# Normalising an attention tile in three passes, each counted, and one wait per transpose round

## The chip, the cores and the metric

The kernel runs on one core of a Trainium2 chip. The metric is the time on the device in microseconds, a median over several runs. The engines of a core run side by side and meet only at semaphores: PE (matmuls and transposes; its weight loads are listed apart as PEld), ACT (activations and copies), DVE (elementwise work and reductions), POOL (elementwise work, here also some DMAs) and SP (issues DMAs).

## What is computed

Three layers follow one another: attention over 16 heads with pooled queries, a mixture of four experts, and a mixture of eight experts with one expert for each token. Only the attention is touched by the change:

```
B, H, S, D = 2, 8, 1152, 64
q_pool = q.reshape(B, H, S // 2, 2, D).mean(axis=3)          # 576 queries a head
scores = scale * q_pool @ k^T                                # 576 x 1152
attn = exp(scores - max(scores))
attn = attn / (sum(attn) + 1e-9)                             # the step that is changed
out = attn @ v                                               # 576 x 64, float32
```

All is float32. To keep accuracy with the faster matmul type, operands are split in a high part (a copy in fp32r) and a low part (the rest), and products are summed over both.

## The kernel before

The 576 queries of a head are cut in five tiles (`QT`): four of 128 queries and one of 64. The 16 heads go by in eight pairs, ten tiles a pair (`TPP = 10`, `TPH = 5`); tile k of pair j has the running number g = 10 j + k, and t = k mod 5 is its place in its head. Pairs 1 to 6 are a loop on each engine, pairs 0 and 7 are written out.

For each tile: PE makes the scores (`score_tile`, L290 and L291, 128 x 1152 in three PSUM banks). DVE takes the negated row maximum (`max_tile`, L745). ACT makes the exponential and the row sum into the SBUF tile `a[t]` (`exp_tile`, L550). DVE adds 1e-9 and takes the reciprocal (`rinv_tile`, L751 and L754). POOL multiplies the whole tile by it, in place, in one instruction of 1152 columns (`norm_tile`, L1021), and raises `norm_ready` by one. PE then transposes the tile in nine blocks of 128 columns, three to a round (`transpose_round`, L307 and L309, `RPT = 3` rounds of `KPR = 3` blocks), each round into one of two PSUM banks (`ring`). ACT copies a round to `aTh` (`split_hi`, L514), DVE subtracts to `aTl` (`split_lo`, L700), and PE multiplies by V (`times_v`, L322) in two groups a head, at t = 3 (first 288 queries) and at the next head's t = 0 (the other 288).

The order is written out by hand in a function `pair` on every engine, by fixed leads: in the stage of tile k PE makes the scores of tile k + 4, ACT the exponential of k + 3, DVE the reciprocal and POOL the multiply of k + 2 (`N_LEAD = 2`), while PE, ACT and DVE transpose and split tile k. PE's order in a stage is: round 0, then `times_v` where it is due, round 1, the scores and round 2 (round 2 before the scores where `times_v` is due).

Beside the tiles, POOL makes the low parts of K and V for later heads: `sub_k` (L1006, 64 x 1152) after the multiply of the stages k = 3 and k = 8, and `sub_v` (L1012, 128 x 576) after that of k = 4 and k = 9. So four POOL instructions stand in a row: the multiply for the next head's tile 0, `sub_k`, the multiply for its tile 1, `sub_v`. SP loads a later head's K, Q and V when `k_lo`, `v_lo` and `q_sum` have risen.

DVE at k = 0 and k = 5 makes, between its splits, the low part of the scaled queries of the next head (`prep_ql`, L738, a SCALAR_TENSOR_TENSOR with both inputs in SBUF), and at k = 5 of pairs 1 to 7 it also splits the last pair's output (`split_x`: L774, a copy `xTh<-y` listed as CAST, and L700, `xTl<-y,xTh`, with two SBUF inputs). In pair 7 there is no `prep_ql` at k = 5 and no `sub_k`.

`at_least(eng, s, v)` is a `wait_ge` that is left out when v is the constant 0. Where an instruction has one wait it carries it; a further wait is an instruction of its own on the engine's queue (EVENT_SEMAPHORE in the trace), and in a loop the value waited for is made by a register operation (ALU_OP).

Of the kernel before, what the change touches and what calls it, by code (L numbers as in the profile page):

```python
# [5 lines left out]
ALU = mybir.AluOpType  # L6
# [6 lines left out]
P = 128  # L13
BATCH, HEADS, SEQ, DH = 2, 8, 1152, 64
POOL = 2
QS = SEQ // POOL
NH = BATCH * HEADS
# [3 lines left out]
TPH = len(QT)  # L21
TPP = 2 * TPH
RPT = 3
KPR = KT_N // RPT
# [29 lines left out]
def attention_moe_moe_kernel(nc, kT, qT, vr, dom, w1, w2, emb, tau, v1, v2, rows, out):  # L54
# [9 lines left out]
    def sb(name, shape, dt=F32, scope=ctx):  # L64
        return scope.enter_context(nc.sbuf_tensor(name, shape, dt))
# [4 lines left out]
    def sem(name):  # L70
        return ctx.enter_context(nc.semaphore(name))
# [3 lines left out]
    def at_least(eng, s, value):  # L75

        if not isinstance(value, int) or value > 0:
            eng.wait_ge(s, value)

    with ctx:  # L80
# [37 lines left out]
        a = [sb(f"a{i}", [P, SEQ], F32, att) for i in range(TPH)]  # L118
# [8 lines left out]
        rinv = sb("rinv", [P, TPH], F32, att)  # L127
# [65 lines left out]
        def bank(turn):  # L193
            return ring[turns.index(turn) % 2]
# [8 lines left out]
        def bank_free(eng, j, turn, first):  # L203

            i = turns.index(turn) - 2
            if first and i == turns.index(("V", 0, 1)):
                i -= 2
            if i >= 0 or not first:
                at_least(eng, *taken(j if i >= 0 else j - 1, turns[i]))
# [10 lines left out]
        S = {n: sem(n) for n in names}  # L220
# [57 lines left out]
        def _(pe):  # L278
# [15 lines left out]
            def transpose_round(t, k, r, j, g, first):  # L294

                m = QT[t][1]
                if r == 0:
                    pe.wait_ge(S["norm_ready"], g + 1)
                bank_free(pe, j, ("T", k, r), first)
                for i in range(KPR):  # L300
                    kt = KPR * r + i
                    o = bank(("T", k, r))[:, i * m:(i + 1) * m]
                    src = a[t][0:m, kt * P:(kt + 1) * P]
                    if m < P and i == 0:


                        last = pe.matmul(o, src, ident[0:m, 0:m], start=True, stop=True)  # L307
                    else:
                        last = pe.transpose(o, src, ident[0:m, 0:m])  # L309
                last.then_inc(S["t_ready"], 1)  # L310
# [46 lines left out]
            def pair(j, first, last):  # L357
                for k in range(TPP):
                    s, t = k // TPH, k % TPH
                    g = TPP * j + k  # L360
                    transpose_round(t, k, 0, j, g, first)
                    if t == 0 and not (first and k == 0):
                        times_v(2 * j + s - 1, 1 - s, 1, j, k, first)
                    if t == V_TILES[0]:
                        times_v(2 * j + s, s, 0, j, k, first)
                    transpose_round(t, k, 1, j, g, first)
                    if t in V_TILES:
                        transpose_round(t, k, 2, j, g, first)
                    if not (last and k + S_LEAD >= TPP):
                        s2, t2 = (k + S_LEAD) // TPH, (k + S_LEAD) % TPH  # L370
                        score_tile(2 * j + s2, s2 % 2, t2, g + S_LEAD)
                    if t not in V_TILES:
                        transpose_round(t, k, 2, j, g, first)
                    if last and k == TPP - 2:
                        pe.wait_ge(S["x_lo"], PAIRS - 1)
                    if last and k >= TPP - 2:

                        for f in range(2 * (k - TPP + 2), 2 * (k - TPP + 2) + 2):
                            up_tile(0, 0, f)
# [601 lines left out]
        def _(pool):  # L981
# [19 lines left out]


            def sub_k(n, s, norms):
                at_least(pool, S["norm_ready"], norms)
                pool.wait_ge(S["k_hi"], n + 1)
                pool.tensor_tensor(KT[s][DH:P, :], rawK[s][DH:P, :], KT[s][DH:P, :].bitcast(F32),  # L1006
                                   ALU.subtract).then_inc(S["k_lo"], 1)

            def sub_v(n, s, norms):
                at_least(pool, S["norm_ready"], norms)  # L1010
                pool.wait_ge(S["v_hi"], n + 1)
                pool.tensor_tensor(VV[s][:, :, DH:2 * DH], rawV[s][:], VV[s][:, :, 0:DH].bitcast(F32),  # L1012
                                   ALU.subtract).then_inc(S["v_lo"], 1)

            def norm_tile(t, g, ks, vs):
                pool.wait_ge(S["k_lo"], ks)
                pool.wait_ge(S["v_lo"], vs)
                at_least(pool, S["norm_ready"], g)
                pool.wait_ge(S["rinv_ready"], g + 1)
                m = QT[t][1]  # L1020
                pool.tensor_tensor(a[t][0:m, :], a[t][0:m, :], rinv[0:m, t:t + 1].to_broadcast([m, SEQ]),  # L1021
                                   ALU.mult).then_inc(S["norm_ready"], 1)


            pool.wait_ge(S["fill_ready"], 1)
# [9 lines left out]
            chain(pool.tensor_scalar(first1[:], prefer[:], float(E2), None, ALU.is_ge))  # L1035

            sub_v(0, 0, 0)
            pool.wait_ge(S["v_lo"], 1)
            pool.wait_ge(S["k_lo"], 1)
            sub_k(1, 1, 0)  # L1040
            for t in range(N_LEAD):
                norm_tile(t, t, 2, 1)
            def pair(j, first, last):
                for k in range(TPP):
                    s, t = k // TPH, k % TPH
                    g = TPP * j + k
                    n = 2 * j + s
                    if not (last and k + N_LEAD >= TPP):
                        norm_tile((k + N_LEAD) % TPH, g + N_LEAD, NH if last else n + 2 + (t > 3),
                                  n + 1)  # L1050
                    if t == V_TILES[0] and not last:
                        sub_k(n + 2, s, g + N_LEAD + 1)
                    if t == 4 and not (last and s == 1):
                        sub_v(n + 1, 1 - s, g + N_LEAD + 1)
# [4 lines left out]
            pair(PAIRS - 1, False, True)  # L1059

            pool.wait_ge(S["x_lo"], PAIRS)
            pool.wait_ge(S["norm_ready"], TPH * NH)
            pool.memset(acc[:], 0.0).then_inc(S["acc_zero"], 1)


# [64 lines left out]
```

## Time and profile before

| | us |
|---|---|
| median of 3 runs | 1005.42 (1002.42 to 1006.47) |
| span of the profiled execution, first to last instruction | 1002.8 |
| median less that span | 2.6 |
| PE busy in the span | 879.9 (88%) |
| DVE busy | 511.9 (51%) |
| ACT busy | 435.0 (43%) |
| POOL busy | 285.1 (28%) |
| loop pairs 1 to 6 and their neighbours, 92 to 348 us | 256.0 |

The record gives the profiled execution its span alone; its whole time on the device is not listed beside the three runs. A row of a timeline gives start, duration, engine, line, operation, output and inputs, shapes and count; the bracket at its end is the idle time of the engine before it and what ended it. Busy engines are not by themselves the limit: in the attention stages the engines hand work on in a ring, and the chain of waits says which hand-over was last.

### The profile page before, as it was taken

Reading aid. Unit: us, or ns where it says so; the run is one execution under the profiler, and the core shown is the slowest. Engines: PE = TensorE matmul, PEld = TensorE weight load, DVE = VectorE, ACT = ScalarE, POOL = GpSimd, SP = SyncE. Lnnn points to the kernel's source line nnn. Section 1 sums busy time; section 2 is a strip of 40 time slices with the busy share of each in tenths; the row PEclk is TensorE's granted clock in tenths of the full one; section 3 lists DMA queues with packets and bytes.
Section 4 is the critical chain, followed back from the end, with each engine's and each line's share of the span. In section 5 each row is a group of like instructions: output and inputs, shape, how many; then the busy total and the mean of one; then the engine's idle time right before and its main releaser. Section 6 shows DMA issues by size and latency. Waiting matters only on the chain.

```text
span 1002.8 us, 14755 instructions
## 1 busy us (share of the span) xinstructions
PE 879.9 (88%) x4740; PEld 753.5 (75%) x4741; DVE 511.9 (51%) x901; ACT 435.0 (43%) x794; POOL 285.1 (28%) x166
## 2 busy tenths in 40 slices
PE   2888888888888879999999999999999709999996
PEld 2666666666666768898989898989898607878885
DVE  4788888888878854141414141314131322299225
ACT  4677777777777643030303031303131502278224
POOL 3766667766667521000000000000000040133112
PEclk9999999999999979999999999999999858999998
DMA  8333222234227221010201120012000062197510
GB/s 263 83 83 84 71 59 59 59 81 95 59 59 185 75 85 52 33 49 37 84 1 32 53 84 0 22 62 84 1 1 1 0 235 70 42 308 255 209 42 23
DMA packets 30095, 79.66 MB, mean 79 GB/s; under 512 B 4008, under 2 KB 4008, under 8 KB 30065
## 3 DMA queue, kind: packets, MB, share of 16 engines
q1 hardware_dynamic: 27104, 70.58, 23.9%
q0 software_dynamic: 2960, 8.68, 2.7%
q8 instruction: 19, 0.31, 0.1%
q14 instruction: 12, 0.09, 0.0%
HBM read 69.52 MB, written 10.78 MB: 80 GB/s over the span
## 4 chain that ended last, share of the span: by engine, by line
PE 76%; ACT 7%; issue 6%; DVE 6%; DMA 3%; POOL 1%; SPq 1%; ACTq 0%; POOLq 0%; DVEq 0%
PE L L337 20%; PE L L400 20%; PE ring L322 7%; PE L L505 7%; PE L L479 6%; PE ring L309 4%; PE scores L290 4%; PE scores L291 3%; ACT a L550 2%; DVE aTl L700 2%; ACT aTh L514 2%; PE ring L307 1%; DMA xr<-sorted_rows 1%; ACT o_vl L514 1%; POOL sorted_rows L1069 1%
## 5 line engine op out<-in xcount | busy, mean ns | idle before, releaser
L1021 POOL TENSOR_TENSOR a<-a,rinv 128x1152 f32<-128x1152 f32 (+1 forms) x80 | 168.5, 2106 | 106.2 <-DVE rinv L754 104.1
L700 DVE TENSOR_TENSOR aTl<-ring,aTh 128x384 fp32r<-128x384 f32 (+1 forms) x240 | 118.5, 512 | 62.0 <-ACT aTh L514 60.6
L309 PE MATMUL ring<-ident,a 128*128 128x128 f32 (+1 forms) x672 | 110.4, 277 | 37.1 <-ACT o_vl L514 18.2
L514 ACT ACTIVATE aTh<-ring 128x384 fp32r<-128x384 f32 (+1 forms) x240 | 106.5, 458 | 70.9 <-PE ring L309 66.3
L619 ACT ACTIVATE hh<-L 128x384 fp32r<-128x384 f32 x96 | 46.6, 491 | 204.2 <-PE L L337 204.2
L337 PE MATMUL L<-xTh,w1h 128*128 128x384 f32 x384 | 131.2, 342 | 4.4 <-DVE hl L832 2.3
L337 PE MATMUL L<-xTl,w1h 128*128 128x384 f32 x384 | 130.8, 341 | 0.0
L337 PE MATMUL L<-xTh,w1l 128*128 128x384 f32 x384 | 130.6, 340 | 0.0
L1069 POOL DMA_INDIRECT sorted_rows<-acc,posi x9 | 10.7, 1186 | 415.0 <-DVE posi L924 412.6
L309 PEld LDWEIGHTS ring<-ident,a 128*128 128x128 f32 (+1 forms) x672 | 75.4, 145 | 64.9 <-DVE aTl L700 32.8
L832 DVE SCALAR_TENSOR_TENSOR hl<-L,hh 128x384 fp32r<-128x384 f32 x96 | 52.8, 557 | 125.4 <-ACT hh L619 125.4
L400 PE MATMUL L<-w2h,hh 128*128 128x512 f32 x288 | 114.2, 396 | 0.0
L400 PE MATMUL L<-w2l,hh 128*128 128x512 f32 x288 | 113.8, 395 | 0.0
L400 PE MATMUL L<-w2h,hl 128*128 128x512 f32 x288 | 113.7, 395 | 0.0
L745 DVE TENSOR_REDUCE negmax<-scores 128x1 f32<-128x1152 f32 (+1 forms) x80 | 107.9, 1350 | 2.2 <-PE scores L291 2.2
L839 DVE SCALAR_TENSOR_TENSOR acc<-L,pw,acc 128x512 f32<-128x512 f32 x36 | 27.0, 751 | 158.7 <-PE L L400 158.7
L290 PE MATMUL scores<-KT,QTh 128*128 128x384 f32 (+1 forms) x240 | 90.6, 378 | 13.8 <-DVE QTl L738 7.8
L550 ACT ACTIVATE a<-scores,negmax 128x1152 f32<-128x1152 f32 (+1 forms) x80 | 97.1, 1214 | 5.3 <-DVE negmax L745 5.3
L322 PE MATMUL ring<-aTh,VV 128*128 128x288 f32 x288 | 81.5, 308 | 19.1 <-DVE aTl L700 19.1
L291 PE MATMUL scores<-KT,QTl 128*128 128x384 f32 (+1 forms) x240 | 83.0, 346 | 0.0
L514 ACT ACTIVATE w2h<-raw 128x1024 fp32r<-128x1024 f32 x40 | 39.5, 1048 | 90.5 <-PE L L400 88.0
L322 PE MATMUL ring<-aTl,VV 128*128 128x288 f32 x288 | 78.5, 298 | 0.0
(155 smaller groups left out, 1580.6 us busy)
## 6 DMA issues: line engine op xcount, KB each, us to landing
raw<-in_v SPq DMA_DIRECT2D x48, 512.0 KB, 5.9
raw<-in_w SPq DMA_DIRECT2D x32, 512.0 KB, 5.2
rawK<-in_kT SPq DMA_DIRECT2D x32, 288.0 KB, 5.1
rawQ<-in_qT SPq DMA_DIRECT2D x32, 288.0 KB, 5.8
sorted_rows<-filler SPq DMA_DIRECT2D x19, 257.0 KB, 9.4
rawV<-in_vr SPq DMA_DIRECT2D x16, 288.0 KB, 5.9
xr<-sorted_rows POOLq DMA_DIRECT2D x15, 257.0 KB, 3.0
out<-o,destc POOLq DMA_INDIRECT x13, 2.8
```

Source lines behind the costliest of these rows:

```text
L290: pe.matmul(o, QTh[s][:, q0:q0 + m], KT[s][:, keys], start=True, stop=False)
L291: last = pe.matmul(o, QTl[s][:, q0:q0 + m], KT[s][:, keys], start=False, stop=True)
L309: last = pe.transpose(o, src, ident[0:m, 0:m])
L322: last = pe.matmul(O[:, 0:w], VV[s][:, kt, :], src[:, kt, q0:q0 + w], start=(kt == 0 and i == 0), stop=(kt == KT_N - 1 and i == 1))
L337: last = pe.matmul(L1[i % L1_BANKS][:, 0:CW], w[:, d, wf], x[:, cols], start=(n == 0), stop=(n == 3 * DT - 1))
L400: last = pe.matmul(L2[tt % L2_BANKS][:], h[c % 2][:, f, cols], w[:, f, :], start=(n == 0), stop=(n == 3 * FT - 1))
L505: last = pe.matmul(L2[1][:], h[:, f, :], w[:, f, :], start=(n == 0), stop=(n == 3 * FT - 1))
L514: return act.activation(o, i, ACT.Copy, **kw)
L550: act.activation(a[t][0:m, :].rearrange("p (c k) -> p c k", c=SC), scores[b][0:m, :, 0:SW], ACT.Exp, bias=negmax[0:m, t:t + 1], accum_out= ...
L700: return dve.tensor_tensor(o, i0, i1, op)
L745: dve.reduce_max(negmax[0:m, t:t + 1], scores[b][0:m, :, 0:SW], axis=AX.XY, negate=True).then_inc(S["max_ready"], 1)
L1021: pool.tensor_tensor(a[t][0:m, :], a[t][0:m, :], rinv[0:m, t:t + 1].to_broadcast([m, SEQ]), ALU.mult).then_inc(S["norm_ready"], 1)
```

## The change

POOL's multiply of a tile is issued as three instructions of 384 columns, in the order of the rounds, each raising `norm_ready` by one. Every transpose round waits for its own count instead of round 0 alone waiting for the whole tile. All other waits on `norm_ready` are scaled by `RPT = 3`, so they wait for the same event as before.

```diff
@@ transpose_round (PE)
-                if r == 0:
-                    pe.wait_ge(S["norm_ready"], g + 1)
+                pe.wait_ge(S["norm_ready"], RPT * g + r + 1)
                 bank_free(pe, j, ("T", k, r), first)
@@ sub_k, sub_v (POOL)
-                at_least(pool, S["norm_ready"], norms)
+                at_least(pool, S["norm_ready"], RPT * norms)
@@ norm_tile (POOL)
-                at_least(pool, S["norm_ready"], g)
+                at_least(pool, S["norm_ready"], RPT * g)
                 pool.wait_ge(S["rinv_ready"], g + 1)
                 m = QT[t][1]
-                pool.tensor_tensor(a[t][0:m, :], a[t][0:m, :], rinv[0:m, t:t + 1].to_broadcast([m, SEQ]),
-                                   ALU.mult).then_inc(S["norm_ready"], 1)
+                for r in range(RPT):
+                    keys = slice(r * KPR * P, (r + 1) * KPR * P)
+                    pool.tensor_tensor(a[t][0:m, keys], a[t][0:m, keys],
+                                       rinv[0:m, t:t + 1].to_broadcast([m, KPR * P]),
+                                       ALU.mult).then_inc(S["norm_ready"], 1)
@@ before the memset of acc (POOL)
-            pool.wait_ge(S["norm_ready"], TPH * NH)
+            pool.wait_ge(S["norm_ready"], RPT * TPH * NH)
```

## Rows read from the trace of the kernel before

**Rows 1.** Busy time by stretch, columns engine by engine, with instructions, clock, DMA.
```profile
92.00:348.00 256.00, 213.61 (x1365) 173.61 (x1365) 213.12 (x401) 190.46 (x382) 175.32 (x84) 1.00 0.34 83
```
**Rows 2.** Waits, 92 to 350 us: engine, line, releaser, total, times, longest.
```profile
POOL a L1021 <- DVE rinv L754: 76.3, 49, 2.8
```
**Rows 3.** Timeline, stage k = 2 of a loop pair: weight loads of transposes, POOL.
```profile
204.98 2.11 POOL L1021 TENSOR_TENSOR a<-a,rinv 128x1152 f32<-128x1152 f32 x1 [2.09 <-DVE rinv L754]
...
208.15 0.31 PEld L309 LDWEIGHTS ring<-ident,a 128*128 128x128 f32 x3 [0.15 <-DVE aTl L700]
```
**Rows 4.** Chain of waits, stage k = 5: start, duration, piece.
```profile
219.26 0.58 ACT QTh L514
...
220.54 1.68 DVE xTh L774
...
222.33 0.76 DVE xTl L700
```
**Rows 5.** Timeline of DVE, stage k = 5.
```profile
219.86 0.76 DVE L738 SCALAR_TENSOR_TENSOR QTl<-qs,QTh 128x576 fp32r<-128x576 f32 x1
220.54 1.66 DVE L774 CAST xTh<-y 128x576 f32 x1
222.33 0.76 DVE L700 TENSOR_TENSOR xTl<-y,xTh 128x576 f32 x1
```
**Rows 6.** Timeline of POOL, the four in a row, and the next multiply.
```profile
212.75 2.11 POOL L1021 TENSOR_TENSOR a<-a,rinv 128x1152 f32<-128x1152 f32 x1 [2.24 <-DVE rinv L754]
215.02 2.64 POOL L1006 TENSOR_TENSOR KT<-rawK,KT 64x1152 fp32r<-64x1152 f32 x1 [0.16 <-POOL a L1021]
217.82 2.11 POOL L1021 TENSOR_TENSOR a<-a,rinv 128x1152 f32<-128x1152 f32 x1 [0.16 <-POOL KT L1006]
220.00 1.88 POOL L1012 TENSOR_TENSOR VV<-rawV,VV 128x576 fp32r<-128x576 f32 x1
223.43 2.11 POOL L1021 TENSOR_TENSOR a<-a,rinv 128x1152 f32<-128x1152 f32 x1 [1.54 <-DVE rinv L754]
```
**Rows 7.** Timeline, stage k = 0: POOL, then DVE behind it.
```profile
198.40 1.42 POOL L1012 TENSOR_TENSOR VV<-rawV,VV 128x576 fp32r<-128x576 f32 x1
...
198.82 1.61 DVE L738 SCALAR_TENSOR_TENSOR QTl<-qs,QTh 128x576 fp32r<-128x576 f32 x1
```
**Rows 8.** Timeline of DVE, first aTl after it in stage k = 0.
```profile
201.23 1.17 DVE L700 TENSOR_TENSOR aTl<-ring,aTh 128x384 fp32r<-128x384 f32 x2 [0.53 <-ACT aTh L514]
```
**Rows 9.** All instructions of line 774: count, shortest/median/longest ns.
```profile
L774 DVE CAST xTh<-y x8: 452/1664/1664, 92.2 to 385.3; 128x576 f32 x6, 128x576 fp32r<-128x576 f32 x2
```
**Rows 10.** times_v at k = 5 and k = 8: chain in pair 0, timeline in a loop pair.
```profile
47.94 2.65 PE ring L322 x18
...
60.24 2.63 PE ring L322 x18
...
218.19 0.40 PE L322 MATMUL ring<-aTh,VV 128*128 128x288 f32 x1 [0.41 <-DVE aTl L700]
...
231.32 0.39 PE L322 MATMUL ring<-aTh,VV 128*128 128x288 f32 x1 [0.78 <-DVE aTl L700]
```
**Rows 11.** Timeline of POOL, small instructions at the start.
```profile
0.42 0.10 POOL L1119 MEMSET const-float32-0.0<- 128x1 f32 x1 [0.42 <-issue]
0.45 0.10 POOL L1119 MEMSET const-float32-1.0<- 128x1 f32 x1
...
4.78 0.24 POOL L1035 TENSOR_SCALAR first<-prefer 128x8 f32<-128x8 f32 x1
```
**Rows 12.** Sequencer work of line 1019, a wait of POOL: ns.
```profile
L1019 POOLq ALU_OP  x60: 32/32/32, 71.6 to 324.4; - x60
L1019 POOLq EVENT_SEMAPHORE  x20: 43/43/43, 24.5 to 357.5; - x20
```
**Rows 13.** Timeline of pair 7, stage k = 5: POOL's sub_v and DVE's copy.
```profile
347.58 1.43 POOL L1012 TENSOR_TENSOR VV<-rawV,VV 128x576 fp32r<-128x576 f32 x1
...
348.08 1.25 DVE L774 CAST xTh<-y 128x576 fp32r<-128x576 f32 x1
```

More of the change, by code:

```diff
@@ L1009, in sub_v @@
             def sub_v(n, s, norms):
-                at_least(pool, S["norm_ready"], norms)
+                at_least(pool, S["norm_ready"], RPT * norms)
                 pool.wait_ge(S["v_hi"], n + 1)
```

## The prediction

> **What bounds the kernel now.** I read the busy shares, then the waits, then the chain, then the timelines of the places where the chain touches POOL. In the loop pairs no engine is full: in 256.0 us PE is busy 213.6, DVE 213.1, ACT 190.5, POOL 175.3 [rows 1]. So the attention is bound by hand-overs between PE, ACT and DVE. POOL is not in that ring as a releaser: among the waits of this stretch it waits for DVE's reciprocal, 49 times, 76.3 us in all [rows 2], and no row has PE or PEld waiting for POOL. The tightest place is stage k = 2 to 3: the multiply of tile 3 runs from 204.98 to 207.09 and its first transposes load at 208.15, released by DVE's aTl [rows 3]. That leaves 1.06 us of slack. At k = 6 it ends at 219.93 [rows 6] and round 0 follows only behind xTl, which ends at 223.09 [rows 5].
>
> There is one place where POOL does reach the chain, by another way. At k = 5 of pairs 1 to 7 the chain runs ACT's QTh copy, DVE's xTh copy (1.68 us), DVE's xTl [rows 4]. That copy takes 0.45 us with POOL idle and 1.66 in the median [rows 9]. In the loop it starts at 220.54, POOL's sub_v ends at 221.88 [rows 6], and the copy ends 0.32 later, at 222.20 [rows 5]. The copy is held until POOL's instruction is over. The same happens to the SCALAR_TENSOR_TENSOR of line 738: 0.76 us where it starts ahead of sub_v [rows 5], 1.61 where sub_v (198.40 to 199.82) is running, ending 0.61 after it [rows 7]. The other way round, sub_v takes 1.42 alone [rows 7] and 1.88 behind line 738 [rows 6]. So these instructions and POOL's take turns at something, and the one that comes second waits.
>
> **The change, part by part.**
>
> Earlier release of round 0, removed wait. Gain 0: round 0 now needs only the first third of a multiply that was ready 1.06 us ahead at its tightest place [rows 3]. The cover is DVE's aTl that frees the bank; rounds 1 and 2 come later still, so a last pass that ends some tenths later is hidden too.
>
> Two more POOL instructions a tile. The trace has no multiply of 384 columns. What a further pass costs: the 1152-column sub_k takes 2.64 and the 576-column sub_v 1.42 [rows 6, 7]; the slope leaves 2.64 - 2 x (2.64 - 1.42) = 0.20 us that does not depend on the columns. An 8-column instruction takes 0.24 and a one-column memset 0.10 [rows 11]. Against that, instructions with no wait between them overlap: the memsets of 0.10 start 0.03 apart [rows 11]. I take 0.20 less some 0.07 of overlap a pass, so a multiply grows by e = 2 x 0.13, say 0.25 us, from 2.11 to 2.36. The lower end is 0: the columns are the same, so less than one instruction's time is excluded, and full overlap gives no more than that. The upper end is a fixed 0.24 with a gap of 0.16 as stands ahead of sub_k [rows 6], e = 0.8.
>
> POOL's busy time rises by 80 x 0.25 = 20 us; nearly all of it falls in idle time before a reciprocal (1.5 to 2.2 us each) [rows 6]. SP's loads start up to 0.5 later, from about 222.1; K is first copied at about 232 and a transfer of this kind lands in some 6 us, so they stay hidden.
>
> The four in a row at k = 3 and 4. Two multiplies, sub_k and sub_v run back to back with gaps of 0.16 and 0.07 [rows 6], so sub_v starts 2e = 0.50 later: 220.50. Line 738 is issued at 219.86. Now the last pass of the multiply (219.66 to 220.43) is running, so it is held 0.5 us and ends near 220.43 + 0.61 = 221.04. Sub_v has waited since 220.50 and goes next; today it ends 1.26 after line 738 does (221.88 against 220.62) [rows 5, 6], so now at 222.30. The copy ends 0.32 later, 222.62, against 222.20: +0.42. All of it goes on through xTl to the splits, since DVE is the chain there [rows 4]. That DVE's work at k = 5 is really paid for shows in the pairs: from times_v of k = 5 to that of k = 8 it takes 12.30 us in pair 0, which has no split_x, and 13.13 in a loop pair [rows 10]. The 0.83 between them is also the most that could be won here.
>
> Six loop pairs: 6 x 0.42 = 2.5 us. Pair 7 has no sub_k and no line 738; there sub_v (347.58) is behind one multiply, moves by e, and the copy, which ends 0.32 after it, moves too [rows 13]: +0.25. At k = 0 the same shift lets line 738 in ahead of sub_v or leaves it behind; it is done by 200.9 at worst, and DVE then had 0.53 idle ahead of its next split [rows 8]. Cost 0.
>
> Here the Trainium skill speaks: its page "SBUF — State Buffer", section "SBUF: two separate sides", says that VectorE and GpSimd share a port pair under an exclusive lock that the first to start holds for the whole instruction, and that VectorE takes it in its two-port modes and also with two SBUF inputs against a GpSimd op that reads SBUF. The first half agrees with the 1.66 against 0.45 us above. The second half would also hold xTl (two SBUF inputs), which no row shows next to a POOL instruction; what hangs on that is the second case below.
>
> 160 more waits on PE, for rounds 1 and 2. The nearest rows are a wait of 43 ns and a register operation of 32 on POOL's queue [rows 12]. All exposed: 160 x 0.075 = 12 us. Behind such a wait stand the round's loads, then ACT's split. I take 0: the count is long reached, and PE's queue is fed while it still works on scores or times_v or stands at a bank. Round 0 carries the same pair of waits today and starts 0.15 us after its release [rows 3]. The upper end is 4 us, one exposed wait in three.
>
> Sum: +2.5 + 0.25 = +2.8 us on a span of 1002.8. The median of the runs is 1005.4, 2.6 above the span, and I add to the median: 1008.2, 0.3% more.
>
> **The rivals.**
>
> A, nothing moves. If the passes overlap fully (e near 0), sub_v stays where it is: 1005.4. For: overlapped starts [rows 11]. Against: those are memsets that read nothing.
>
> B, faster: DVE slips in between passes. With e over about 0.43 (0.5, say) the last pass would start after line 738 is issued; line 738 goes between passes two and three and ends near 220.7, the last pass ends at 221.35 and the copy, already waiting, goes ahead of sub_v and ends at 221.67. If xTl is not held by POOL it ends at 222.56 instead of 223.09, -0.53 in six pairs; in pair 7 the copy wins against sub_v and saves 0.8: 1005.4 - 4.0 = 1001.4. If xTl is held, it waits for sub_v to end near 222.97 and the pair loses 0.5 again. Against it: line 738, with two SBUF inputs, is held [rows 7], and e must be double my value. With the 0.83 of [rows 10] in seven pairs it can't go below 999.6.
>
> C, slower: passes cost 0.97 us each, e = 0.8. Then the last pass runs to about 222.0, sub_v after the copy to 223.75, and xTl, held, to 224.36 instead of 223.09: 6 x 1.27 + 0.8 = 8.4, 1013.8. It decides at the four in a row, from e of about 0.5 on. For: the 0.24 of an instruction with 8 columns. Against: the 0.20 of the slope.
>
> D, slower: PE's waits show, up to 4 us on top of 2.8: 1012.2. Against: round 0's start today.
>
> **How the numbers follow.** Forecast (1008.2, e of 0.1 to 0.45) 0.54; A 0.14; B 0.12; C 0.12; D 0.08. A measurement of this kernel can tell about 0.5%, 5 us, from no change. B is at most 6 us, so three quarters of it count as faster: 0.09. C and D count as slower: 0.20. The rest, 0.71, is within. The range leaves out the end of B below 1001.5 and the worse part of C above 1012.5.
>
> **What would show it.** A pass should take 0.75 to 0.85 us and a multiply 2.3 to 2.5 from first start to last end. PE should wait nowhere for POOL. In the loop pairs sub_v should start about 0.5 later behind its reciprocal, line 738 at k = 5 take about 1.2 instead of 0.76, and the copy still end 0.3 after sub_v. From times_v of k = 5 to k = 8 should come 13.5 instead of 13.13, and the rest of a pair stay. I am wrong if the copy goes ahead of sub_v, if the gaps ahead of rounds 1 and 2 grow, or if the expert stages move.

## The result, and the profile after

The changed kernel takes 1009.7 us in the median of 10 runs (1007.9 to 1010.9), against 1005.2 of the kernel before in the same session. The ratio is 1.0047, 95% interval 1.0034 to 1.0059: slower by 4.5 us (3.4 to 5.9), where the prediction had 2.8.

The page of the changed kernel, its head. POOL has 160 instructions more and is 27.1 us longer busy (24.3 in the multiplies, 2.7 in sub_v; forecast 20). No other engine has more work, but PE's queue has 195 waits and register operations more, which the page doesn't count as busy.

```profile
span 1006.6 us, 15170 instructions
...
PE 879.1 (87%) x4740; PEld 752.0 (75%) x4741; DVE 510.2 (51%) x901; ACT 435.1 (43%) x794; POOL 312.2 (31%) x326
```

Most of the loss is in the loop pairs. Below are the first times_v instructions of k = 0, 3, 5, 8 and of the next pair's k = 0, in the timeline of the changed kernel (start, duration, engine, line, operation; in brackets the idle time before). The rows that answer to the third and the fourth are the last two of [rows 10].

```profile
200.34 0.40 PE L321 MATMUL ring<-aTh,VV 128*128 128x288 f32 x1 [0.42 <-DVE aTl L699]
...
212.88 0.37 PE L321 MATMUL ring<-aTh,VV 128*128 128x288 f32 x1 [0.89 <-DVE aTl L699]
...
221.48 0.37 PE L321 MATMUL ring<-aTh,VV 128*128 128x288 f32 x1 [0.43 <-DVE aTl L699]
...
235.26 0.37 PE L321 MATMUL ring<-aTh,VV 128*128 128x288 f32 x1 [0.80 <-DVE aTl L699]
...
243.85 0.40 PE L321 MATMUL ring<-aTh,VV 128*128 128x288 f32 x1 [0.42 <-DVE aTl L699]
```

The same of the kernel before, at k = 0, 3 and the next 0; k = 5 (218.19) and k = 8 (231.32) are the rows named above.

```profile
197.16 0.40 PE L322 MATMUL ring<-aTh,VV 128*128 128x288 f32 x1 [0.42 <-DVE aTl L700]
...
209.57 0.39 PE L322 MATMUL ring<-aTh,VV 128*128 128x288 f32 x1 [0.88 <-DVE aTl L700]
...
239.95 0.40 PE L322 MATMUL ring<-aTh,VV 128*128 128x288 f32 x1 [0.42 <-DVE aTl L700]
```

| stretch, us | before | changed | difference |
|---|---|---|---|
| k = 0 to 3 | 12.41 | 12.54 | +0.13 |
| k = 3 to 5 | 8.62 | 8.60 | -0.02 |
| k = 5 to 8 | 13.13 | 13.78 | +0.65 |
| k = 8 to 0 | 8.63 | 8.59 | -0.04 |
| a loop pair | 42.79 | 43.51 | +0.72 |

Six pairs make 4.3 us; from the first of them at k = 3 to the same place in pair 7 it is 4.5 (256.6 before, 261.1 changed). The rest of the spans' difference of 3.8 us is small and of both signs: by the same starts, 0.56 before the first times_v of k = 3, 0.50 in pair 0, and then -1.0 in the last pair and -0.7 in the experts. The 0.56 can't be put down to the change: in the profiled executions of all nine kernels this first stretch takes 39.3 to 41.2 us, and experiment 5, which has the code of before there, takes 40.97. The -1.0 is probably no merit of the change either. These are the stretches from pair 7's k = 3 to the last times_v (time, then busy times, then the granted clock, DMA share and GB/s). The first row is before, the second after. The profiled execution of before spent more of it at the lower of the two clock levels, 1.2 GHz (0.88 of full speed in the mean, against 0.92), and PE took 1.2 us longer over the same 188 instructions. That the clock makes the whole difference is not shown: the kernel of experiment 6 takes 41.0 there at 0.92.

```profile
337.85:379.32 41.47, 33.20 (x188) 28.87 (x189) 23.65 (x43) 20.49 (x42) 13.06 (x7) 0.88 0.16 52
```

```profile
343.40:383.84 40.44, 32.00 (x188) 27.64 (x189) 24.20 (x43) 20.50 (x42) 15.73 (x18) 0.92 0.16 53
```

**POOL and DVE at k = 5.** The timeline of the changed kernel; it answers to [rows 5 and 6].

```profile
218.60 2.64 POOL L1005 TENSOR_TENSOR KT<-rawK,KT 64x1152 fp32r<-64x1152 f32 x1 [0.16 <-POOL a L1022]
...
221.40 2.40 POOL L1022 TENSOR_TENSOR a<-a,rinv 128x384 f32<-128x384 f32 x3 [0.16 <-POOL KT L1005]
...
223.13 1.28 DVE L737 SCALAR_TENSOR_TENSOR QTl<-qs,QTh 128x576 fp32r<-128x576 f32 x1
...
223.88 1.80 POOL L1011 TENSOR_TENSOR VV<-rawV,VV 128x576 fp32r<-128x576 f32 x1
...
224.34 1.66 DVE L773 CAST xTh<-y 128x576 f32 x1
...
226.12 0.76 DVE L699 TENSOR_TENSOR xTl<-y,xTh 128x576 f32 x1
```

Three passes take 2.40 us together where one took 2.11. Line 737 (738 before) is now issued while the last pass runs and takes 1.28 instead of 0.76; before, it was issued 0.07 before the multiply ended and so hardly waited. It ends 0.61 after the last pass; sub_v waits for it; the copy is held until sub_v ends at 225.68 and ends 0.32 later, as before. Counted from times_v of k = 5, xTl ends at 5.40 (226.88 - 221.48) instead of 4.90 (223.09 - 218.19): +0.50.

**PE's waits.** The timeline of the kernel before, one freed bank at k = 7: aTl ends at 227.75, the weight load starts at 227.80.

```profile
227.19 0.56 DVE L700 TENSOR_TENSOR aTl<-ring,aTh 128x384 fp32r<-128x384 f32 x1 [0.44 <-ACT aTh L514]
...
227.80 0.31 PEld L309 LDWEIGHTS ring<-ident,a 128*128 128x128 f32 x3 [0.95 <-DVE aTl L700]
```

The same place in the changed kernel: aTl ends at 231.60, the load starts at 231.72.

```profile
231.04 0.56 DVE L699 TENSOR_TENSOR aTl<-ring,aTh 128x384 fp32r<-128x384 f32 x1 [0.50 <-ACT aTh L513]
...
231.72 0.31 PEld L308 LDWEIGHTS ring<-ident,a 128*128 128x128 f32 x3 [1.01 <-POOL a L1022]
```

Take the transposes' loads between 92 and 348 us that PE waited for and that start less than 160 ns after the end of an aTl: the median distance went from 53 ns (67 loads) to 116 (83 loads). The sequencer's records of line 78, the function that waits for a bank, show why. Before (from 92 to 348 us; count, duration in ns):

```profile
L78 PEldq ALU_OP  x163: 32/32/36, 93.4 to 322.2; - x163
...
L78 PEldq EVENT_SEMAPHORE  x10: 51/51/51, 324.0 to 346.4; - x10
```

After:

```profile
L78 PEldq EVENT_SEMAPHORE  x168: 51/51/51, 92.6 to 347.0; - x168
L78 PEldq ALU_OP  x66: 32/32/36, 92.8 to 327.7; - x66
```

Of the two waits of a round, the first-written one (the count, long reached) is now carried by the weight load, and the bank's, which really ends last, has become an instruction of 51 ns in front of it. The trace lists the semaphore of each wait and bears this out: between 92 and 318 us the transposes' loads carry the wait on `norm_ready` 130 times in the changed kernel and never before, and the register operations that carried it before (53 times, round 0's) carry it 26 times. The bracket "<-POOL a L1022" in the row at 231.72 is a trap: the load carries the wait on POOL's count, and so the record names POOL. Wherever it does so, the tile's last pass had ended at least 1.9 us before. From 92 to 350 us the changed kernel's list of waits puts 16.3 us (25 waits) down to POOL for the loads of line 308 and 3.0 us (12 waits) for those of line 306, and none of it is time that POOL cost.

### The profile page after: what moved, and what is told of

The parts are those of the page before. It is cut to its first block, busy times and chain, and to the rows that moved or that the text cites. A ratio compares the mean times of both kernels' runs of the same rounds, so it can differ in the third digit from the quotient of the medians.

```text
span 1006.6 us, 15170 instructions
## 1 busy us (share of the span) xinstructions
PE 879.1 (87%) x4740; PEld 752.0 (75%) x4741; DVE 510.2 (51%) x901; ACT 435.1 (43%) x794; POOL 312.2 (31%) x326
## 4 chain that ended last, share of the span: by engine, by line
PE 78%; DVE 7%; ACT 5%; issue 5%; DMA 3%; POOL 1%; SPq 1%; ACTq 0%; POOLq 0%; DVEq 0%
PE L L336 20%; PE L L399 20%; PE L L504 7%; PE ring L321 6%; PE L L478 6%; PE ring L308 6%; PE scores L290 5%; PE scores L291 4%; DVE aTl L699 3%; ACT aTh L513 2%; PE ring L306 1%; DMA xr<-sorted_rows 1%; POOL sorted_rows L1071 1%; PE L L486 1%; DVE xTh L773 1%
## 5 line engine op out<-in xcount | busy, mean ns | idle before, releaser
L1022 POOL TENSOR_TENSOR a<-a,rinv 128x384 f32<-128x384 f32 (+1 forms) x240 | 192.8, 831 | 85.8 <-DVE rinv L753 81.9
```

The costliest lines, as they stand in the source:

```text
L1022: pool.tensor_tensor(a[t][0:m, keys], a[t][0:m, keys], rinv[0:m, t:t + 1].to_broadcast([m, KPR * P]), ALU.mult).then_inc(S["norm_ready"], 1)
```

## The experiments

The theory has two parts: POOL's longer multiply pushes sub_v and with it DVE's copy (the port part, after the port pair that the prediction cites for the two engines' taking turns), and the bank's wait now costs an instruction on PE (the wait part). The rivals are either of them alone.

**1. PE's waits alone.** One multiply as before, all else as in the change.

```diff
-                for r in range(RPT):
-                    ...
+                pool.tensor_tensor(a[t][0:m, :], a[t][0:m, :], rinv[0:m, t:t + 1].to_broadcast([m, SEQ]),
+                                   ALU.mult).then_inc(S["norm_ready"], RPT)
```

> One multiply of 1152 columns as before, raising the count by 3; PE waits in every transpose round as in the change. Theory 1 (two causes: the port shift through POOL's longer multiply, and a wait instruction on PE's queue that now stands between the freed bank and the transposes): a round starts 0.12 us after DVE's aTl instead of 0.05, a loop pair takes 42.79 + 0.20 to 0.25 us, the copy xTh ends where it did; about +1.5 to +2 us in all. Theory 2 (POOL alone): a loop pair stays at 42.79 and the time at that of before. Theory 3 (PE's waits alone are the whole loss): a pair takes 43.5 and the time is +4.5.

Measured: 1007.7 against 1004.7, ratio 1.0027 (1.0016 to 1.0037). The five times_v starts of its timeline, k = 0, 3, 5, 8, 0:

```profile
200.16 0.40 PE L321 MATMUL ring<-aTh,VV 128*128 128x288 f32 x1 [0.41 <-DVE aTl L699]
...
212.70 0.37 PE L321 MATMUL ring<-aTh,VV 128*128 128x288 f32 x1 [0.89 <-DVE aTl L699]
...
221.31 0.37 PE L321 MATMUL ring<-aTh,VV 128*128 128x288 f32 x1 [0.42 <-DVE aTl L699]
...
234.62 0.37 PE L321 MATMUL ring<-aTh,VV 128*128 128x288 f32 x1 [0.80 <-DVE aTl L699]
...
243.21 0.39 PE L321 MATMUL ring<-aTh,VV 128*128 128x288 f32 x1 [0.41 <-DVE aTl L699]
```

A pair takes 43.05, +0.26: 0.13 in k = 0 to 3, 0.18 in k = 5 to 8, and a few hundredths less in the other two. That is four times the 0.06 by which a round starts later; for the other rounds of a pair it doesn't show. The median distance from aTl to load is 115 ns. Waits alone cost, so theory 2 falls. The medians differ by 3.0 us (1.6 to 3.7), above the expected 1.5 to 2; the trace has 2.1 of it between pair 0's k = 3 and pair 7's.

**2. POOL's passes alone.** The change with PE waiting once a tile.

```diff
-                pe.wait_ge(S["norm_ready"], RPT * g + r + 1)
+                if r == 0:
+                    pe.wait_ge(S["norm_ready"], RPT * (g + 1))
```

> Three passes of 384 columns as in the change, but PE waits once for all three, in round 0 alone, as before. Theory 1: sub_v starts 0.58 us later, xTl ends 0.50 later, a loop pair takes 42.79 + 0.50 = 43.3, with all of it between times_v of k = 5 and of k = 8; rounds start 0.05 after DVE's aTl; +3 us. Theory 2: all of the loss, a pair at 43.5, +4.5. Theory 3: nothing.

Measured: 1007.3, ratio 1.0029 (1.0017 to 1.0042). Its times_v starts at k = 0, 3, 5, 8, 0:

```profile
198.58 0.39 PE L322 MATMUL ring<-aTh,VV 128*128 128x288 f32 x1 [0.41 <-DVE aTl L700]
...
210.98 0.40 PE L322 MATMUL ring<-aTh,VV 128*128 128x288 f32 x1 [0.88 <-DVE aTl L700]
...
219.62 0.40 PE L322 MATMUL ring<-aTh,VV 128*128 128x288 f32 x1 [0.41 <-DVE aTl L700]
...
233.23 0.40 PE L322 MATMUL ring<-aTh,VV 128*128 128x288 f32 x1 [0.79 <-DVE aTl L700]
...
241.85 0.39 PE L322 MATMUL ring<-aTh,VV 128*128 128x288 f32 x1 [0.41 <-DVE aTl L700]
```

A pair takes 43.27, +0.48, all of it between k = 5 and k = 8 (13.61); k = 0 to 3 stays at 12.40, and the distance from aTl to load is back at 53 ns. The two parts add up: 0.26 + 0.48 = 0.74 a pair, against 0.72 in the changed kernel. PE here waits for the last pass in round 0, and nothing is late for want of an earlier count: in the loop pairs round 0 starts 0.7 us or more after its tile's last pass. The medians can't show this sum: +3.0 and +2.6 make 5.6 against 4.5, with intervals of some 1 us to either side of each. It rests on the times_v starts, which agree from one loop pair to the next within 0.04 us.

**3. The waits in the other order.**

```diff
-                pe.wait_ge(S["norm_ready"], RPT * g + r + 1)
                 bank_free(pe, j, ("T", k, r), first)
+                pe.wait_ge(S["norm_ready"], RPT * g + r + 1)
```

> The changed kernel with the two waits of a transpose round written in the other order, the bank first and the count second. If the delay on PE comes from which wait is carried by the weight load and which is an instruction of its own ahead of it, the bank's wait now is carried, rounds start 0.05 us after DVE's aTl again, and a loop pair takes 43.3 instead of 43.5: about -1.5 us against the change. If the delay comes from the number of wait and register instructions, it stays at 43.5.

Measured: 1008.4, ratio 1.0037 (1.0022 to 1.0051). Half of the expectation came. In pair 0, where the counts are constants, the median distance is 53 ns again and k = 5 to 8 takes 12.32, against 12.52 in the changed kernel and 12.30 before. These are its times_v pieces of pair 0 in the chain of waits (k = 5 and 8), to set beside the first two of [rows 10]:

```profile
48.20 2.65 PE ring L321 x18
...
60.52 2.62 PE ring L321 x18
```

In the loop it didn't help: 123 ns and 43.66 in the pair from 200.11, no better than 43.51. The sequencer's records of line 298, the count's wait, say how:

```profile
L298 PEldq ALU_OP  x110: 32/32/32, 92.1 to 329.3; - x110
L298 PEldq FUSED_REGOPS  x54: 37/37/51, 96.5 to 327.1; - x54
L298 PEldq EVENT_SEMAPHORE  x13: 51/51/51, 329.7 to 347.1; - x13
```

In the loop the count's value is made by a register operation, which stands between the two waits; in the records that operation itself carries the bank's wait, and the load comes behind it, so the freed bank still has another instruction to release first. So it is not the number of waits but which instruction the last-ending one sits on.

**4. Nine passes.** POOL's part in a larger dose, PE waiting once.

```diff
-                for r in range(RPT):
+                for c in range(KT_N):
                     ...                                 # 128 columns each
```

> Nine passes of 128 columns, PE waiting once in round 0 as before: a larger dose of the POOL part. A pass more costs 0.145 us by the change (2.40 against 2.11), so a multiply should take 2.11 + 8 x 0.145 = 3.27. Port theory: two multiplies push sub_v by 2.3 us; line 738 slips in between passes, and xTl, if two SBUF inputs are held too, ends about 1 to 2.3 later, a pair at 43.8 to 45.1, +7 to +15 us. If the loss were a fixed cost of having more instructions, or if DVE gets through between short passes and xTl is not held, a pair takes 43.3 or less.

Measured: 1029.8, ratio 1.0253 (1.0235 to 1.0271). A multiply takes what was expected:

```profile
223.29 3.25 POOL L1023 TENSOR_TENSOR a<-a,rinv 64x128 f32<-64x128 f32 x9 [0.16 <-POOL a L1023]
```

The time is 25.1 above before, beyond the expected end of +15. The waits of the stretch from 92 to 380 us have a row that no smaller dose had:

```profile
PE ring L309 <- POOL a L1023: 31.5, 21, 2.7
```

Here the wait is real and the multiply binds: at k = 2, 6 and 7 of every loop pair, and at 3 and 8 of most, round 0 starts 0.13 us after its tile's last pass. The 1.06 us of slack at round 0 [rows 3] are used up when a multiply is 1.14 longer and late by the one before it. The port part didn't grow with the dose, it turned round. These are the multiply of k = 4 and DVE at k = 5, where times_v starts at 233.63:

```profile
234.40 4.52 POOL L1023 TENSOR_TENSOR a<-a,rinv 128x128 f32<-128x128 f32 x9 [0.16 <-POOL KT L1006]
...
235.31 0.82 DVE L738 SCALAR_TENSOR_TENSOR QTl<-qs,QTh 128x576 fp32r<-128x576 f32 x1
236.05 0.65 DVE L774 CAST xTh<-y 128x576 f32 x1
236.82 0.76 DVE L700 TENSOR_TENSOR xTl<-y,xTh 128x576 f32 x1
```

DVE gets in between the short passes and ahead of sub_v. The copy takes 0.65 instead of 1.66, and xTl ends 3.95 after times_v instead of 4.90, while the multiply is stretched to 4.52 and PE waits for it. So this run says where the slack ends and what short passes do to the order of the two engines, and doesn't measure the port part of three passes.

**5. The kernel before, with DVE's split of the output moved from k = 5 to k = 8**, where POOL is idle.

```diff
-                    if k == TPH and not first:
-                        split_x(j - 1)
                     if t not in V_TILES:
                         split_lo(t, k, g, 1)
+                    if k == TPH + V_TILES[0] and not first:
+                        split_x(j - 1)
                     if not (last and k + N_LEAD >= TPP):
```

> The kernel before with the split of the last pair's output (xTh, xTl) moved in DVE's order from stage k = 5 to k = 8, ahead of the reciprocal, where POOL waits for that reciprocal and so is idle. If the copy's wait behind sub_v is what makes k = 5 long, the copy takes 0.45 us, xTl 0.76, and times_v of k = 5 to k = 8 falls from 13.13 to pair 0's 12.30; DVE had 1.5 us idle at k = 8, so that stage grows by little. Up to 0.83 x 7 = -5.8 us, about 999. If the 0.83 is plain DVE work, it only moves to k = 8 and the time stays at 1005.

Measured: 1000.1 against 1004.4, ratio 0.9953 (0.9937 to 0.9968). All eight copies are short now (shortest, median and longest in ns), which answers to [rows 9]:

```profile
L774 DVE CAST xTh<-y x8: 444/453/455, 106.0 to 380.6; 128x576 f32 x6, 128x576 fp32r<-128x576 f32 x2
```

The times_v starts at k = 0, 5, 8, 0:

```profile
196.33 0.40 PE L322 MATMUL ring<-aTh,VV 128*128 128x288 f32 x1 [0.42 <-DVE aTl L700]
...
217.34 0.40 PE L322 MATMUL ring<-aTh,VV 128*128 128x288 f32 x1 [0.41 <-DVE aTl L700]
...
229.65 0.40 PE L322 MATMUL ring<-aTh,VV 128*128 128x288 f32 x1 [0.78 <-DVE aTl L700]
...
238.27 0.39 PE L322 MATMUL ring<-aTh,VV 128*128 128x288 f32 x1 [0.41 <-DVE aTl L700]
```

k = 5 to 8 takes 12.31, pair 0's time, k = 8 to 0 still 8.62, and a pair 41.94 instead of 42.79. So the copy's place cost 0.85 a pair in the kernel before too. The median fell by 4.3 us, where up to 5.8 had been expected; this version is faster than both kernels.

**6. The changed kernel with the same move.**

> The changed kernel with the same move. Port theory: sub_v may come 0.58 later at no cost now, since the copy no longer stands behind it, so the POOL part (0.48 a pair) is gone and only PE's part (0.26 a pair) is left: a loop pair 0.26 above split_at_8, about 1.5 to 2 us slower than that kernel in all. If the longer multiply costs by itself and not through the copy, the distance to split_at_8 stays at 0.73 a pair, 4.5 us.

Measured: 1001.7, ratio 0.9970 (0.9959 to 0.9982). Its times_v starts at k = 0 and the next pair's k = 0:

```profile
196.35 0.39 PE L321 MATMUL ring<-aTh,VV 128*128 128x288 f32 x1 [0.42 <-DVE aTl L699]
...
238.51 0.40 PE L321 MATMUL ring<-aTh,VV 128*128 128x288 f32 x1 [0.42 <-DVE aTl L699]
```

A pair takes 42.16, 0.22 above experiment 5, with 0.13 and 0.12 of it in k = 0 to 3 and 5 to 8: the wait part alone. The longer multiply (2.40, and 2.91 once a pair, where line 737 is held and then runs between two passes) costs nothing that shows in k = 5 to 8 once the copy is gone from behind sub_v. The port part is thereby shown by its removal. Over all six pairs the mean difference is 0.30, since k = 3 to 5 took 0.1 to 0.3 longer in three of them, which was not taken apart.

In this kernel, unlike in the changed one, an earlier count is used. The multiply of tile 2 comes late, and its round 0 starts before the last pass is over, at 203.94 against 204.03:

```profile
201.63 2.40 POOL L1022 TENSOR_TENSOR a<-a,rinv 128x384 f32<-128x384 f32 x3 [0.25 <-POOL VV L1011]
...
203.94 0.31 PEld L308 LDWEIGHTS ring<-ident,a 128*128 128x128 f32 x3 [0.16 <-issue]
```

With one count a tile it would start some 0.2 later, by the 0.13 that experiment 4 has from last pass to load; this is an estimate.

**7. The sum of the query halves under sub_k**, in the kernel before: `prep_qs` moved behind round 1's split at k = 3 and 8.

> The kernel before with the sum of the two query halves (qs, a TENSOR_TENSOR of 128 x 576 with two SBUF inputs) moved behind round 1's split at k = 3 and 8, so that it is issued while POOL's multiply or sub_k runs. If POOL holds such an instruction as it held line 738, the sum takes 1.5 to 3 us instead of 0.75, ending about 0.6 after POOL's. If two SBUF inputs alone don't make it wait, it stays at 0.75. This decides what case B of the prediction assumed of xTl.

One run, 1041.2. The timeline at k = 3: POOL's sub_k ends at 214.18, the sum at 214.81, 0.63 later.

```profile
211.55 2.63 POOL L1006 TENSOR_TENSOR KT<-rawK,KT 64x1152 fp32r<-64x1152 f32 x1 [0.16 <-POOL a L1021]
...
211.87 2.94 DVE L700 TENSOR_TENSOR qs<-rawQ 128x576 f32<-128x576 f32 x1
```

At k = 8 the sum started first (190.21, 0.75 us), and sub_k, issued behind it, took 2.99. So a TENSOR_TENSOR with two SBUF inputs is held by POOL, and holds it. The Trainium skill's page "SBUF — State Buffer", section "SBUF: two separate sides", states this rule: a VectorE instruction with two SBUF inputs and a GpSimd instruction that reads SBUF need the same port pair, and the one that starts first has it for its whole instruction. Here the trace agrees in both directions (0.75 to 2.94 us for the sum, 2.64 to 2.99 for sub_k). No run here sets such an instruction beside one of POOL that reads no SBUF. What made this run 36.8 us slower (a pair takes 47.8) was not taken apart.

## Why the prediction was right, and where a size was off

**What bounds it.** Right. The copy behind sub_v is the place where POOL touched the chain, and experiments 5 and 6 show it by taking it away. The smallest slack is 1.01 us, at k = 7, and not the 1.06 read at k = 3; nothing hung on that.

**Gain 0 from the earlier count.** Right for this kernel: experiment 2 has the late count and loses nothing by it. Experiment 6 shows a place where the count would be used.

**The cost of a pass.** e, the growth of a multiply, was taken as 0.25 and is 0.29 (2.40 against 2.11), a pass 0.83 us (forecast 0.75 to 0.85). The fixed 0.20 less 0.07 of overlap was near; what a further pass costs is 0.145.

**The shift at the four in a row.** Right in mechanism and nearly in size: 0.42 a pair forecast, 0.48 measured alone. Line 738 was forecast at about 1.2 and took 1.28; the copy ended 0.32 after sub_v. With e of 0.29 the same working gives 0.50 for the end of the copy, which is what the timeline has. Pair 7's +0.25 shows at xTl, which ends 0.28 later behind times_v, but not in the pair's time, where the last stretch went the other way by 1.0.

**160 waits on PE.** This is the term that was off: "I take 0". It measured 0.26 a pair, some 1.6 us in the loop; in pair 0 another 0.3, by the times_v starts of the changed kernel and of experiment 3 (k = 3 to 5 takes 8.70 and 8.60, k = 5 to 8 takes 12.52 and 12.32). Two steps of the argument failed. It read "starts 0.15 us after its release" from [rows 3], but the bracket gives PE's idle time before the load; the aTl that released it ended 0.06 before, and so the row showed the fast form of the hand-over. And it took round 0 to carry "the same pair of waits": in the loop round 0's count was checked by the register operation ahead and the load carried the bank's wait. The change turned that round, too: all rounds start 0.06 later, not only the 160 with a new wait. Pair 0 loses more (0.43 in experiment 1, from k = 3 to k = 3, against 0.26), and there round 0 had the slow form already before the change; so the cost lies with the new waits of rounds 1 and 2, and that round 0's turn costs anything is not shown. The price is not a queue that is busy with waits, as case D had it, but the hand-over itself. Its size lies between the forecast's 0 and D's 4. The prediction had named this as a sign of being wrong, "if the gaps ahead of rounds 1 and 2 grow", and they grew; so k = 5 to 8 takes 13.78, where 13.5 was forecast, and k = 0 to 3 didn't stay.

**The rivals.** A (passes overlap fully) is out by 2.40 against 2.11. B needed xTl free of POOL and e above 0.43; experiment 7 shows that such an instruction is held, and e was 0.29. B's mechanism exists all the same: with nine passes DVE did get in between. C needed e of 0.8 for three passes and is out by 0.29; the nine passes, 1.14 longer, don't test it, since there the copy no longer stood behind sub_v. D was right in sign.

Together: 6 x (0.48 + 0.26) = 4.4, and the medians moved by 4.5. That these agree so closely is partly luck: pair 0 adds 0.5, and the stretches before and behind the pairs differ from execution to execution by more than that.

## What to carry to other kernels

Before an instruction is split to release its reader earlier, look whether the reader ever waits for it; if not, only the costs are left. Where two engines take turns at a port, look at what starts behind what: a longer instruction far upstream can push the one that a short copy has to wait for, and moving that copy to a stage where the other engine is idle was worth 0.5% here, while the earlier counts brought nothing. Where an instruction has two waits, see in the trace which one it carries: here the hand-over was shortest with the wait that ends last on the instruction itself, and nothing between, register operations included.

## What the runs showed of the hardware

- From the end of the aTl that frees a bank to the weight load it took 53 ns in the median where the load carries the wait, 116 where the wait is an instruction in front of it, and 123 where a register operation carries it (experiment 3).
- A TENSOR_TENSOR with two SBUF inputs took 2.94 us instead of 0.75 behind POOL's sub_k, and lengthened sub_k from 2.64 to 2.99 when it came first.
- POOL's back-to-back passes cost 0.14 to 0.145 us each beyond their columns, for 3 passes (2.40) as for 9 (3.25).
- DVE gets in between POOL's back-to-back instructions: against nine passes of 128 columns a copy took 0.65 us instead of 1.66 behind sub_v, and the nine passes took 4.52 instead of 3.26.
